# Router logits computed with the tokens as the stationary operand, and the routing steps behind them one slot earlier

## The reference

```python
def _moe2_ref(x, w_gate, w1, w2):          # x 1152x512, w_gate 512x8, w1 8x512x1024, w2 8x1024x512
    logits = x @ w_gate
    logits = logits - logits.max()
    P = np.exp(logits)
    for _ in range(8):
        P /= P.sum(1, keepdims=True) + 1e-09
        P /= P.sum(0, keepdims=True) + 1e-09
        P *= N / E
    out = np.zeros((N, D))
    for e in range(E):
        h = np.maximum(x @ w1[e], 0.0)
        out += P[:, e:e + 1] * (h @ w2[e])
    return out
```

## Time and profile before

| what | value |
|---|---|
| median of 3 runs | 1104.81 us (1101.69 to 1104.89) |
| profiled execution, its own time | 1104.89 us |
| its span, first to last instruction | 1103.1 us |
| TensorE busy | 1088.6 us, 99% of the span |
| mean granted TensorE clock | 0.975 of full |
| VectorE, ScalarE, GpSimd busy | 58%, 34%, 3% |

### The profile page before, as it was taken

How to read it: one execution, slowest core, us unless ns; L and a number is a source line. 1 busy time by engine, 2 the same in 40 slices (tenths; PEclk the granted TensorE clock), 3 DMA queues, 4 the chain that set the end, 5 groups by cost and what they waited for, 6 DMA issues and landing times.

```text
span 1103.1 us, 17767 instructions
## 1 busy us (share of the span) xinstructions
PE 1088.6 (99%) x6970; PEld 999.8 (91%) x6970; DVE 644.3 (58%) x1112; ACT 375.8 (34%) x607; POOL 34.4 (3%) x36
## 2 busy tenths in 40 slices
PE   8989999999999999999999999999999999999998
PEld 5879999999998988998998899899889889989987
DVE  5676665556558875664475375557437636644742
ACT  2336664344324431332242142223223313322321
POOL 3440000000000000000000000000000000000000
PEclk7569999999999999999999999999999999999999
DMA  7353112222230210120030021012002101200111
GB/s 185 111 181 87 64 43 68 77 77 67 72 109 21 77 39 20 58 77 20 19 106 27 0 85 48 19 53 80 19 19 76 39 18 57 76 19 19 38 38 48
DMA packets 30225, 64.98 MB, mean 59 GB/s; under 512 B 12396, under 2 KB 14700, under 8 KB 30188
## 3 DMA queue, kind: packets, MB, share of 16 engines
q1 hardware_dynamic: 30188, 64.47, 18.8%
HBM read 62.10 MB, written 2.36 MB: 58 GB/s over the span
## 4 chain that ended last, share of the span: by engine, by line
PE 95%; DVE 3%; DMA 1%; issue 1%; ACT 1%; SPq 0%; DVEq 0%
PE ps L1140 56%; PE ps L1420 31%; PE ps L1212 2%; PE ps L1167 2%; PE ps L1181 1%; PE ps L1217 1%; DMA kt<-kT 1%; PE ps L1229 1%; PE ps L1161 1%; PE ps L1192 0%; DVE w_lo L707 0%; DVE x_lo L707 0%; DVE xf L904 0%; SPq L343 0%; DVE h L1074 0%
## 5 line engine op out<-in xcount | busy, mean ns | idle before, releaser
L1140 PE MATMUL ps<-w_hi,h_hi 128*128 128x512 f32 x576 | 224.4, 390 | 0.0
L1140 PE MATMUL ps<-w_lo,h_hi 128*128 128x512 f32 x576 | 224.2, 389 | 0.0
L1140 PE MATMUL ps<-w_hi,h_lo 128*128 128x512 f32 x576 | 224.2, 389 | 0.0
L642 ACT ACTIVATE h_hi<-h 128x1024 fp32r<-128x1024 f32 (+1 forms) x80 | 77.2, 975 | 253.7 <-PE ps L1140 218.2
L1020 DVE SCALAR_TENSOR_TENSOR acc<-ps,prob_e,acc 128x512 f32<-128x512 f32 x63 | 47.3, 750 | 190.6 <-PE ps L1140 190.6
L1420 PE MATMUL ps<-x_hi,w_hi 128*128 128x288 f32 x512 | 151.2, 295 | 1.0 <-DVE x_lo L707 1.0
L1420 PE MATMUL ps<-x_hi,w_lo 128*128 128x288 f32 x512 | 150.8, 294 | 0.0
L1420 PE MATMUL ps<-x_lo,w_hi 128*128 128x288 f32 x512 | 150.6, 294 | 0.0
L1140 PEld LDWEIGHTS ps<-w_hi,h_lo 128*128 128x128 f32 x576 | 108.1, 188 | 22.4
L1140 PEld LDWEIGHTS ps<-w_lo,h_hi 128*128 128x128 f32 x576 | 108.1, 188 | 22.2
L1140 PEld LDWEIGHTS ps<-w_hi,h_hi 128*128 128x128 f32 x576 | 108.1, 188 | 22.0
(11 more groups left out here) (133 smaller groups left out, 1757.7 us busy)
## 6 DMA issues: line engine op xcount, KB each, us to landing
raw<-w SPq DMA_DIRECT2D x64, 512.0 KB, 3.5
raw<-w_up SPq DMA_DIRECT2D x24, 512.0 KB, 3.6
raw<-w_out SPq DMA_DIRECT2D x16, 384.0 KB, 2.9
vw<-v SPq DMA_DIRECT2D x10, 252.0 KB
qt<-qT SPq DMA_DIRECT2D x4, 576.0 KB, 5.3
kt<-kT SPq DMA_DIRECT2D x4, 576.0 KB, 6.4
v<-v SPq DMA_DIRECT2D x8, 288.0 KB
out<-acc SPq DMA_DIRECT2D x9, 256.0 KB, 2.0
```

What stands on the lines that cost most here:

```text
L642: nc.scalar.activation(h2_hi[:, idx % 2, f0:f1, :], h2[:, f0:f1, t * P:(t + 1) * P], ACT.Relu).then_inc(h2_hi_ready, 1)
L1140: done = nc.tensor.matmul(dst, a, b, start=first and n == 0, stop=last and n == len(terms) - 1)
```

## The change

The logits are computed with the operands swapped. For each of nine tiles of 128 tokens, 8 matmuls have a 128x128 block of tokens as weights and the 16 route columns moving. The result is token by expert at once, in bank 7. The copy on ACT, the nine transposes and two semaphores go. `largest_logit` moves from step 4 to step 3 on DVE, the transpose of the maxima from 5 to 4 and the spreading of the maximum from 7 to 6 on TensorE. DVE's `top_logit` stays at step 6.

```diff
                     if routing and g == 0:
                         act.wait_ge(logits_made, 1)
-                        nc.scalar.copy(h2[0:2 * E, NF2 - 1, :].rearrange("p (c j) -> p c j", j=MC),
-                                       ps[0:2 * E, LOGIT_BANK:LOGIT_BANK + 4, 0:MC]).then_inc(logits_out, 1)
...
-                dve.wait_ge(logits_ready, 1)
+                dve.wait_ge(logits_made, 1)
...
-                if n == 4:
+                if n == 3:
                     largest_logit()
...
-                for c in range(2 * B):
-                    terms = [(route[:, k].rearrange("p i e -> p (i e)"), part[:, k, c * MC:(c + 1) * MC])
+                for t in range(NTT):
+                    terms = [(part[:, k, t * P:(t + 1) * P], route[:, k].rearrange("p i e -> p (i e)"))
                              for k in range(KD) for part in (x_hi, x_lo)]
                     for n, (a, b) in enumerate(terms):
-                        last = nc.tensor.matmul(ps[0:2 * E, LOGIT_BANK + c, 0:MC], a, b,
+                        last = nc.tensor.matmul(ps[:, ROUTE_BANK, t * 2 * E:(t + 1) * 2 * E], a, b,
                                                 start=n == 0, stop=n == len(terms) - 1)
                 last.then_inc(logits_made, 1)
-
-            def transpose_logits():
-                pe.wait_ge(logits_out, 1)
-                for t in range(NTT):
-                    last = nc.tensor.transpose(ps[:, ROUTE_BANK, t * 2 * E:(t + 1) * 2 * E],
-                                               h2[0:2 * E, NF2 - 1, t * P:(t + 1) * P], ident[0:2 * E, 0:2 * E])
-                last.then_inc(logits_ready, 1)
...
-                if n == 2:
-                    transpose_logits()
-                if n == 5:
+                if n == 4:
                     top_logits_row()
-                if n == 7:
+                if n == 6:
                     spread_top()
```

More of the change, by code:

```diff
@@ L207, in build @@
         logits_made = sem("logits_made")
-        logits_out = sem("logits_out")
-        logits_ready = sem("logits_ready")
         top_local = sem("top_local")
@@ L252, in build @@
         DOWN_BANKS = [6, 0, 1, 4, 5, 2, 3, 7, 6]
-        ROUTE_BANK, LOGIT_BANK = 7, 4
+        ROUTE_BANK = 7
         def bank(u):
```

## The result

The changed kernel takes 1113.49 us (median of 5 runs, 1111.33 to 1116.13) against 1104.81 before (5 runs, 1101.69 to 1106.66): the ratio is 1.0087, with a 95% interval from 1.0068 to 1.0106. The two medians differ by 8.7 us, where 7.9 were forecast (1112.8 us). All 32 runs of the changed kernel, these five among them, have a median of 1114.5 us, and the ratio of 1.0087 amounts to 9.6 us (7.5 to 11.7). Its profiled execution has 1115.4 us, with a span of 1113.6.

The account below looks back on a forecast made before the run. TensorE's matmul stream was taken as the bound. P4 later by 7.0 us (slow loads, fallen clock) plus 0.9 us for the moved steps gave +7.9 us on 1104.89, 1112.8 us; range 1105.5 to 1115.5.

Parts of the forecast that it names:

- The bound: Behind the attention, TensorE's single stream of matmuls carries the end; anything added to it or delaying it moves the end equally.
- The copy and the transposes worth nothing: Before P4 in expert 0's routing: both lie beside DVE's work, so removing them leaves P4 at 351.66.
- rival 4: Casts, not DVE, hold P4, so the shorter dependency gains at most 1.0 us less 0.9; 0.06 with anything else.
- 0.11 us per load, taken from the column sum: Swapped logits: 72 loads take 7.9 us at full clock, moving P4 by 2.55 us.
- Rival 2: Swapped logits: loads run at the transposes' 0.07 us, P4 stays, only +0.9 us remains, 1105.8; chance 0.10.
- rival 3: Swapped logits: loads do not overlap (0.19 us) and double when the clock falls, +20 us, 1125; chance 0.03.
- The clock falls inside the burst: Swapped logits: thin 16-column matmuls drop TensorE to 1.2 GHz, P4 moves by 7.0 us in all; chance 0.61.
- Rival 1: Swapped logits: the clock holds through the burst with 0.11 us per load, +3.4 us, 1108.3; chance 0.20.
- When it falls and returns: Clock falls 3.1 us into the burst (1.5 to 4.7), returns about 1.3 us after dense matmuls begin; P3 takes 2.5.
- a rise 1 or 2 us later adds up to 1 us: P3 and P4 after the burst: allowance for the clock returning later than taken, up to 1 us more.
- The moved steps: Routing steps one step earlier: spreading behind P7 costs 1.1 us more, the hole behind P5 saves 0.2, together +0.9 us.
- Sum: Whole kernel: +7.0 and +0.9 give +7.9 us on 1104.89, so 1112.8 us, +0.7%.

Follow-up runs that it names:

- experiment 5: The kernel before without the copy and the nine transposes, logits computed as before; P4 started 7.63 us after the first logit matmul, as before.
- experiment 3: The changed kernel with each of the 72 small matmuls moving its 16 columns 15 times over (240 columns); 1108.99 us, ratio 1.0022 to the kernel before.
- bursts of four, six and nine tiles: The changed kernel (nine) and versions computing logits for only four or six tiles; P4 14.97, 7.61 and 9.65 us after the first logit matmul, respectively.
- experiment 1: The changed kernel with the three moved routing steps back in their old places (4, 5, 7); 1113.86 us, ratio 1.0074 to the kernel before.
- experiment 6: The changed kernel with DVE's top_logit also one step earlier (5); stretch from first logit matmul to P2 of group 1 25.1 us, 1.1 less than the changed kernel's.
- the split kernel: The changed kernel with its 72 small matmuls in three bursts of 24 behind P1, P2 and P3; 1114.92 us, ratio 1.0102 to the kernel before.

## Why the prediction was right

- **The bound.** Right: TensorE's stream carries the end, and the stretch's 9.04 us stand between the 8.7 us of the medians and the 9.6 us of the ratio.
- **The copy and the transposes worth nothing.** Right: experiment 5 shows it, and rival 4 falls with it.
- **0.11 us per load, taken from the column sum.** Right: 0.111 at full clock, and 0.114 with 240 columns. Rival 2's 0.07 and rival 3's 0.19 are out. Without the clock's fall these loads moved P4 by 2.98 us (2.55 forecast). The 81 ns of the Trainium skill (TensorE: Matmul & The Clock Gate, section "Back-to-back issue gap") are not what these loads need.
- **The clock falls inside the burst.** Right, and it is the largest term. Of the 9.04 us, experiment 3 gives back 5.3. The attention's matmuls that the prediction calls 65 to 126 columns wide also had some of 144 and of 252 (bf16) columns among them, all wider still than 16, so the comparison stands. Rival 1, by which an occupied TensorE keeps its clock, is refuted for 16-column matmuls. So is the literal reading of the Trainium skill (same page, section "Why this matters for your kernels"): the changed kernel's window has TensorE busy for 7.90 of 7.90 us at 0.50.
- **When it falls and returns.** Partly off. The fall came 3.7 us in, counted from the first load as in the prediction (3.1 taken, 1.5 to 4.7 as bounds), and the low loads take 0.213 us (0.21). The return was mis-sized: 1.3 us after the dense matmuls had begun was read from one place, and it took 5.3. So all of P3 ran slow (3.0 us, 2.5 forecast), and most of P4, which had no term (+0.93); "a rise 1 or 2 us later adds up to 1 us" did not reach that far. P4's start moved by 7.3 us (7.0 forecast), and that this is so close is partly luck: the later fall shortened the burst by 0.2 to 0.3 us, and against that the slow P3 took 0.5. The trace of the kernel before had a second, slower return that the prediction did not use. Its 512-column warm-up matmuls begin at 8.39, the clock still falls at 8.8, and it is back only at 12.25, 3.9 us after they began:

```profile
8.39 3.38 PE L1265 MATMUL ps<-ones 128*128 128x512 f32 x4
```

```profile
8.50:9.00 0.50, 0.50 (x1) 0.84 1.17 296
...
12.00:12.50 0.50, 0.50 (x8) 0.75 0.25 101
```

- **The moved steps.** +0.9 forecast, +0.77 in the changed kernel and +0.8 alone. The wait for `top` behind P7 is 1.04 us (1.1 forecast), the one behind P5 0.32 (0.4 to 0.5).
- **Sum.** 7.9 forecast, 9.0 in the trace, 8.7 between the medians, 9.6 by the ratio. What is short is the late return of the clock: P4's 0.93 us and P3's 0.5.

Without the clock's fall, the rest of the sum was 3.4 us forecast; experiment 3 has 3.7 in the stretch. Counted from the first small matmul, the clock fell after 2.3, 3.8 and 3.6 us in the bursts of four, six and nine tiles, which start alike, and after 3.9 and 3.5 us in the same nine tiles of experiments 1 and 6. Why it differs stays open; no run here varied that alone.

## What to carry to other kernels

Before swapping the operands of a narrow product, count weight loads, not flops: 72 loads of 128 columns cost 8 us at the full clock where 32 passes over 288 columns cost 4.2, and the copy and transposes that the swap saves may be hidden. Look at what else the narrow stream does: at 16 columns per load TensorE fell to 1.2 GHz, even in a burst of 4.5 us, and the next 4 to 6 us of dense work were slow too. When a chain that alternates between two engines is pulled one step earlier, all of its links must move, or the pulled one waits for the one left behind.

## What the runs showed that I had not expected

- The clock fell inside four small tiles (2.3 us in, with the last matmul at 4.3), and, in the split kernel, 0.6 us after dense work had begun again. It returned 4.6 and 5.3 us after dense matmuls had begun in the kernels of four and of nine tiles (353.1 and 362.7 against 348.5 and 357.4); over all kernels with the swapped logits in one narrow burst it was 4.0 (six tiles) to 6.0 us (experiment 1).
- A useless widening made the kernel 4.5 us faster than the narrow one (1108.99 against 1113.49, with the kernel before at 1104.66 and 1104.81 beside them).
- The first logit matmul starts anywhere from 342.1 to 346.7 us in the executions profiled here, though the code ahead of it is the same. That is up to 4.5 us of spread in a kernel whose runs differ by as much. A change below 3 us shows in the stretch of a trace and not in the median.
